# First head: row 1's turns and splits in another order; row 0 restacked first, expert weights in pieces

## The reference

```python
q_pool = q.reshape(B, H, S // 2, 2, D).mean(axis=3)        # B 2, H 8, S 1152, D 64
scores = (1.0 / np.sqrt(D)) * np.matmul(q_pool, k.transpose(0, 1, 3, 2))
scores = scores - np.max(scores, axis=-1, keepdims=True)
attn = np.exp(scores)
attn = attn / (np.sum(attn, axis=-1, keepdims=True) + 1e-09)
out = np.matmul(attn, v)

# x is attn_out as (1152, 512); 8 experts, each token goes to the one with the largest logit
h = np.maximum(x[mask] @ w1[e], 0.0)                        # w1 (8, 512, 1024)
out[mask] = gate_w[mask, None] * eom[mask, e, None] * (h @ w2[e])

h = x @ w_in                                                # w_in (512, 2048)
g = h * np.tanh(np.log1p(np.exp(h)))
return (g @ w_out).astype(np.float32)
```

## Time and profile before

| | |
|---|---|
| median of 3 runs | 677.72 us (677.46 to 678.32) |
| profiled execution | 679.0 us, of which the span shown is 677.3 |
| busy | PE 98%, DVE 75%, ACT 60%, POOL 14% |
| granted clock, mean | 0.998 |
| DMA | 93.83 MB, 139 GB/s over the span |

### The profile page before, as it was taken

One profiled execution on the slowest core, in us unless ns is written; L12 is line 12 of the kernel. 1 busy time (PEld: TensorE's weight loads), 2 busy tenths in 40 slices (PEclk: granted clock), 3 DMA queues, 4 the chain that ended last, 5 costly groups with the idle time before them and its releaser, 6 DMA issues.

```text
span 677.3 us, 14740 instructions
## 1 busy us (share of the span) xinstructions
PE 664.0 (98%) x5135; PEld 591.9 (87%) x5135; DVE 504.9 (75%) x1180; ACT 409.7 (60%) x839; POOL 92.0 (14%) x136
## 2 busy tenths in 40 slices
PE   8999999999999999999999999999999999999996
PEld 6889898988898999579999999899998988899995
DVE  5777677777777776676666676676999998887873
ACT  5767576666666666554656475666676655445542
POOL 7705040505041200220000000000000000101001
PEclk9999999999999999999999999999999999999999
DMA  8888869797977600469990752041200000001001
GB/s 182 186 274 211 249 146 259 181 261 176 264 172 204 150 2 9 174 244 395 398 367 16 279 199 83 15 156 54 86 1 1 1 0 1 32 16 47 1 0 47
DMA packets 95351, 93.83 MB, mean 139 GB/s; under 512 B 41920, under 2 KB 70976, under 8 KB 94784
## 3 DMA queue, kind: packets, MB, share of 16 engines
q1 hardware_dynamic: 91536, 84.39, 42.8%
q10 hardware_dynamic: 2320, 4.00, 1.9%
q0 software_dynamic: 1440, 4.72, 1.8%
HBM read 59.80 MB, written 16.78 MB: 113 GB/s over the span
## 4 chain that ended last, share of the span: by engine, by line
PE 81%; SPq 6%; DVE 5%; POOL 2%; issue 2%; ACT 2%; DMA 0%; ACTq 0%; DVEq 0%; POOLq 0%
PE score_banks L1161 14%; PE score_banks L1191 11%; PE score_banks L1176 10%; PE pvT L902 9%; PE turn L922 9%; PE score_banks L1213 4%; PE pvT L1213 4%; PE turn L1213 4%; PE score_banks L873 4%; PE score_banks L874 4%; SPq L560 2%; PE score_banks L879 1%; PE turn L823 1%; PE turn L1139 1%; PE turn L1148 1%
## 5 line engine op out<-in xcount | busy, mean ns | idle before, releaser
L1261 ACT ACTIVATE prob<-score_banks,nmax 128x1152 f32<-128x1152 f32 x72 | 88.0, 1222 | 51.8 <-DVE nmax L1527 51.8
L922 PE MATMUL turn<-ident,prob 128*128 128x128 f32 x648 | 102.4, 279 | 0.5 <-DVE probT L1583 0.5
L1161 PEld LDWEIGHTS score_banks<-xsT,w_slot 128*128 128x128 f32 x832 | 94.6, 192 | 2.2 <-issue 1.4
L1161 PE MATMUL score_banks<-xsT,w_slot 128*128 x832 | 95.2, 276 | 0.7 <-ACT xsT L1395 0.7
L1266 ACT ACTIVATE probT<-turn 128x384 f32<-128x384 f32 x144 | 69.9, 487 | 36.7 <-PE turn L922 36.7
L922 PEld LDWEIGHTS turn<-ident,prob 128*128 128x128 f32 x648 | 75.1, 141 | 15.0 <-issue 11.0
L902 PE MATMUL pvT<-probT,v_sb 128*64 128x128 f32 (+1 forms) x1404 | 85.9, 269 | 0.0
L902 PEld LDWEIGHTS pvT<-probT,v_sb 128*64 128x64 f32 x1404 | 69.5, 137 | 11.9 <-issue 11.9
L873 PE MATMUL score_banks<-kT,qT 128*128 128x384 f32 x192 | 70.7, 368 | 1.7 <-DMA kT<-k_lo 1.2
L1748 DVE TENSOR_TENSOR w_lo<-w_slot,w_hi 128x512 fp32r<-128x512 f32 x104 | 69.2, 689 | 3.3 <-ACT w_hi L1421 3.2
L1517 DVE TENSOR_REDUCE nmax_part<-score_banks 128x1 f32<-128x768 f32 x72 | 68.3, 949 | 2.0 <-PE score_banks L874 1.8
(11 more groups left out here) (261 smaller groups left out, 1332.8 us busy)
## 6 DMA issues: line engine op xcount, KB each, us to landing
w_slot<-moe_w SPq DMA_DIRECT2D x16, 2048.0 KB, 15.4
slots_dram<-zeros SPq DMA_DIRECT2D x8, 1472.0 KB, 11.6
raw_k<-k SPq DMA_DIRECT2D x16, 288.0 KB, 6.0
v_sb<-v SPq DMA_DIRECT2D x16, 288.0 KB, 4.6
w_in_sb<-moe_w_in SPq DMA_DIRECT2D x2, 2048.0 KB, 7.7
w_out_sb<-moe_w_out SPq DMA_DIRECT2D x2, 2048.0 KB, 9.3
raw_q<-q SPq DMA_DIRECT2D x14, 256.0 KB, 3.4
qT<-q_hi SPq DMA_DIRECT2D x28, 128.0 KB, 2.4
```

The lines of the kernel that those rows point to most:

```text
L922: last = pe.transpose(bank[:, j * P:(j + 1) * P], prob[:, s % 2, c * KC + j * P:c * KC + (j + 1) * P], ident[:, :])
L1161: last = pe.matmul(h1_bank[f % 4][:, 0:P], w1_e[:, d, f * P:(f + 1) * P], xsT[:, d, bass.ds((t % XS_RING) * P, P)], start=(d == 0), stop=( ...
L1261: act.activation(prob[:, s % 2, :].rearrange("p (c n) -> p c n", c=NC), scores[s % 2][:, :, 0:KC], ACT.Exp, bias=nmax[:, s:s + 1], accum_o ...
```

## The change

Four things are moved; two warming matmuls are removed. No other arithmetic is added or taken away.

1. TensorE, first head: the ninth tile's turn goes ahead of the second score product, the turns of row 1's keys go one place back, the query turns are halved around the first scores of tile 1, and the warming matmuls (`WARM_FIRST`) and two waits ahead of the loop go.
2. ScalarE and VectorE, first head: the copies follow the new order of turns, the one of the last key chunk goes behind the first exponential; VectorE splits the last queries of row 0 ahead of tile 1's first maximum.
3. GpSimd, first head: the first pair of row 1's queries is split ahead of the last key chunk; the step that reads a part waits for it by name.
4. SyncE: `restack` sends what row 0 needs first (four query DMAs, six key DMAs) and row 1 behind it; the expert weights go from between `restack(1)` and `load_kq(3)` to the ends of iterations 1, 2 and 3, one matrix each, the gates to that of iteration 4.

```diff
-        first_whole = [("k", 1, 1, 1), ("k", 1, 2, 2), ("q", 0, (FT, Q0), 3), ("k", 1, 0, 4), ("q", 1, (0, FT), 5)]
+        first_whole = [("q", 0, (FT, Q0), 1), ("k", 1, 1, 2), ("k", 1, 2, 3), ("k", 1, 0, 4), ("q", 1, (0, FT), 5)]
...
             def restack(h):
                 par = h % 2
                 sp.wait_ge(q_split, h)
-                for b in range(B):
...
+                restack_queries(0, par, 0, FT * P)
+                for c in range(NC):
+                    sp.wait_ge(k_split, NC * (h - 1) + c + 1)
+                    restack_keys(0, par, c * KC, KC)
+                restack_queries(1, par, Q0 * P, FT * P)
                 for var, q_part in enumerate((q_hi, q_lo)):
                     sp.dma_start(qT[:, par, var, FT * P:Q0 * P].bitcast(F32), q_part[:, FT * P:].bitcast(F32)
                                  ).then_inc(stacked[1], 16)
-                for c in range(NC):
-                    sp.wait_ge(k_split, NC * (h - 1) + c + 1)
-                    restack_keys(0, par, c * KC, KC)
                 restack_keys(1, par, 0, S)
...
             restack(1)
-            for n, w in enumerate((w_gate, w_ogate)):
...
-            load_expert(0, 0)
...
                 if h == 1:
-                    load_w1(1, 1)
+                    load_w1(0, 0)
                     sp.wait_ge(zeros_ready, 1)
                 else:
+                    if h == 2:
+                        load_w2(0, 0)
+                    elif h == 3:
+                        load_w1(1, 1)
+                    elif h == 4:
+                        load_gates()
                     for n in range(2 * (h - 2), min(2 * (h - 1), ZERO_PARTS)):
...
-            first_keys_split(WHOLE_CHUNK0, 3)
-            first_queries_split(WHOLE_Q, 4, (0, FT // 2))
-            first_queries_split(WHOLE_Q, 5, (FT // 2, FT))
-            first_queries_split(WHOLE_TAIL, 6, (FT, Q0))
+            first_queries_split(WHOLE_Q, SPLIT_PAIR0, 1, (0, FT // 2))
+            first_keys_split(WHOLE_CHUNK0, SPLIT_CHUNK0)
+            first_queries_split(WHOLE_Q, SPLIT_PAIR1, 2, (FT // 2, FT))
+            first_queries_split(WHOLE_TAIL, SPLIT_TAIL, 3, (FT, Q0))
...
             qk(0, 0)
+            first_tail()
+            pe.wait_ge(first_ready, FIRST_CHUNK2)
+            qk(0, 1)
             pe.wait_ge(first_k_landed[1], 16)
             whole_keys(1)
-            pe.wait_ge(first_ready, FIRST_CHUNK2)
-            qk(0, 1)
-            whole_keys(2)
             pe.wait_ge(first_ready, FIRST_CHUNK0)
             qk(0, 2)
-            first_tail()
+            whole_keys(2)
             whole_keys(0)
-            whole_queries()
+            whole_queries((0, FT // 2))
             pe.wait_ge(first_copied, WHOLE_CHUNK2)
             qk(1, 0)
-            pe.wait_ge(first_copied, WHOLE_TAIL)
             qk(1, 1)
-
-            pe.wait_ge(first_copied, WHOLE_CHUNK0)
-            for m in range(WARM_FIRST):
-                pe.matmul(turn[0][0:DH, 0:P], ident[:, 0:DH], ident[:, :], start=True, stop=True)
+            whole_queries((FT // 2, FT)).then_inc(whole_turned, 1)
             bodies(pe, pe_body)
...
-            for unit in first_units[:-1]:
+            for unit in first_units:
                 first_high(unit)
-            first_high(first_units[-1], (0,))
-            first_copy(first_whole[0])
-            first_high(first_units[-1], (1,))
-            for unit in first_whole[1:-1]:
-                first_copy(unit)
+            for n in (WHOLE_TAIL, WHOLE_CHUNK1, WHOLE_CHUNK2):
+                first_copy(first_whole[n - 1])
             exp(0, 0)
-            first_copy(first_whole[-1])
+            for n in (WHOLE_CHUNK0, WHOLE_Q):
+                first_copy(first_whole[n - 1])
             bodies(act, act_body)
...
             max_first(0, 0)
             max_rest(0, 0)
+            first_low(FIRST_CHUNK0)
             max_first(1, 1)
-            first_low(FIRST_CHUNK0)
             bodies(dve, dve_body)
```

More of the change, by code:

```diff
@@ L423, in build @@
         warm_bank = score_banks[:, 2, :]
-        WARM_BEFORE, WARM_BETWEEN, WARM_FIRST = 12, 3, 2
+        WARM_BEFORE, WARM_BETWEEN = 12, 3
         FIRST_Q, FIRST_TAIL = NC, NC + 1
@@ L586, in restack_keys, with restack_queries @@
                              ).then_inc(stacked[b], 16)
+            def restack_queries(b, par, at, n):
+                src = slice(b * DH, (b + 1) * DH)
+                for var in range(2):
+                    hi, lo = slice(var * DH, (var + 1) * DH), slice((1 - var) * DH, (2 - var) * DH)
+                    sp.dma_start(qT[hi, par, var, at:at + n].bitcast(F32), q_hi[src, 0:n].bitcast(F32)
+                                 ).then_inc(stacked[b], 16)
+                    sp.dma_start(qT[lo, par, var, at:at + n].bitcast(F32), q_lo[src, 0:n].bitcast(F32)
+                                 ).then_inc(stacked[b], 16)
             def restack(h):
@@ L620, in load_w2, with load_gates @@
                              ).then_inc(w_landed[n], 16)
+            def load_gates():
+                for n, w in enumerate((w_gate, w_ogate)):
+                    sp.dma_start(w_both[:, :, n * NE:(n + 1) * NE], w.rearrange("(t p) e -> p t e", p=P)
+                                 ).then_inc(wg_landed, 16)
             def load_expert(e, n):
@@ L706, in first_keys_split, with first_queries_split @@
                 pool.wait_ge(first_split, done)
-            def first_queries_split(n, done, tiles):
+            def first_queries_split(n, done, moved, tiles):
                 unit = ("q", first_whole[n - 1][1], tiles, 0)
@@ L716, in first_queries_split @@
                 pool.tensor_tensor(qT[here, 0, 1, cols], raw, high, ALU.subtract).then_inc(first_low_done, 1)
-                pool.wait_ge(first_low_done, done - SPLIT_KEYS)
+                pool.wait_ge(first_low_done, moved)
                 pool.tensor_copy(qT[there, 0, 1, cols], high).then_inc(first_moved, 1)
-                pool.wait_ge(first_moved, done - SPLIT_KEYS)
+                pool.wait_ge(first_moved, moved)
                 pool.tensor_copy(qT[there, 0, 0, cols], qT[here, 0, 1, cols].bitcast(F32)).then_inc(first_split, 1)
@@ L840, in first_queries, with whole_queries @@
                 last.then_inc(first_turned, 1)
-            def whole_queries():
-                for i in range(FT):
+            def whole_queries(tiles):
+                for i in range(*tiles):
                     last = pe.matmul(first_bank[FIRST_Q][DH:2 * DH, i * P:(i + 1) * P], q_pair[:, 0, i, 1, :], ident[:, :],
                                      start=True, stop=True)
-                last.then_inc(whole_turned, 1)
+                return last
             def first_tail():
@@ L947, in pe_body @@
                     pe.wait_ge(exp_done, g + 1)
+                    if first and s + 1 == FT:
+                        pe.wait_ge(first_split, SPLIT_CHUNK0)
                     if not (final and s == SB - 1):
@@ L1341, in first_high @@
                     act.wait_ge(first_ready, 1)
-                if 0 in parts:
-                    act.activation(qT[here, 0, 0, cols], src, ACT.Copy, scale=QS)
-                if 1 in parts:
-                    act.activation(qT[there, 0, 1, cols], src, ACT.Copy, scale=QS).then_inc(first_hi_ready, 1)
+                act.activation(qT[here, 0, 0, cols], src, ACT.Copy, scale=QS)
+                act.activation(qT[there, 0, 1, cols], src, ACT.Copy, scale=QS).then_inc(first_hi_ready, 1)
             def first_copy(unit):
```

14 lines of the change are left out of this document (6 added, 8 removed).

## The result

The changed kernel took 684.3 us (median of 4 executions, 682.09 to 684.77) against 678.02 for the kernel before on the same chip (4 executions, 677.46 to 679.63): a ratio of 1.0085, interval 1.007 to 1.010. The forecast was 680.0 with a range up to 682.3, so the direction was right and the size too small. The same kernel was measured twice more later (e1 and e12): 682.4, ratio 1.007 (1.0057 to 1.0082), and 681.95, ratio 1.006 (1.0043 to 1.0076). All 16 executions together have a median of 682.15 and run from 680.89 to 684.77; the first four were on the high side.

The account below looks back on a forecast made before the run. TensorE, busy 98%, was taken as the bound, so only its holes could move: - 0.9 - 1.5 + 1.2 + 3.4 + 0.1 = + 2.3 us on the profiled 679.0 is 681.3, less 1.3 for the median 680.0; range 675.3 to 682.3.

Parts of the forecast that it names:

- The first head: Reordered start on the compute engines: step 1 begins 0.9 us sooner, bounds 0.3 and 1.2.
- the splits: GpSimd's reordered splits in the first head: TensorE's cover stays, so they cost nothing.
- the wait ahead of head 2: TensorE's 1.22 us idle before head 2's first key product goes, a gain of 1.5 us with restart.
- the queue as the new bound: SyncE's DMA queue, with the weights in new places, brings keys for heads 4 and 5 later than TensorE asks.
- waits at heads 4 and 5: TensorE idles for keys 1.1 us ahead of head 4 and 3.3 ahead of head 5.
- the landing: Row 0's last key DMA lands 2.3 us after its issue, bounds 2.2 and 3.3.
- my sum of 681.3: Profiled execution of 679.0 us plus the terms' total of 2.3, before conversion to the median.
- the price of a matrix: A 2 MB expert matrix in SyncE's queue adds 5.6 us, bounds 5.2 and 6.1.
- rival B: No change: a matrix costs SyncE's queue only 3.9 to 4.9 us, giving 676.6 to 678.5; chance 0.22.
- Rival C: TensorE loses granted clock near head 5, in a hole of over 3 us, giving 683.6; chance 0.05.
- the high bounds: Matrix 6.1, long issue 0.6 and landing 3.3 together make the sum + 4.9 us.
- Long issues in restack 4: A first DMA issue into SyncE's full queue may take 1.22 instead of 0.60; half, 0.3 us, allowed.

Follow-up runs that it names:

- e1: The changed kernel again, no edit: 682.4 us, ratio 1.007.
- e12: The changed kernel a third time, no edit: 681.95 us, ratio 1.006.
- e8: The kernel before with only the new restack order, row 0 first, on SyncE: 677.5 us.
- e3: The changed kernel with gates and both expert matrices put back ahead of restack 2, the next behind it: 676.72 us, ratio 0.9983.
- e5: The changed kernel with the second and third matrix and the gates moved behind the last restack: 676.69 us, ratio 0.9984.
- e2: The kernel before with only the expert weights and gates in their new places: 683.98 us, ratio 1.0094.
- e4: The changed kernel with 12 transposes of the identity ahead of the wait for the first tile of heads 4 and 6: 684.24 us.
- e7: The kernel before with only the first head's new order on the four compute engines: 677.99 us.
- e10: The kernel of e9 with 14 transposes of the identity ahead of the wait for head 2's first tile: 681.69 us.
- e9: The kernel of e3 with the next matrix moved from behind restack 2 to ahead of it: 683.36 us.

## Why the prediction was wrong

**Right.** The first head (0.9 forecast, 0.8 by e8 less e3); the splits at no cost (e3); the wait ahead of head 2 gone; the queue as the new bound, with waits at heads 4 and 5 and none later; the landing (2.3, measured 2.2 between 135.15 and 137.34). Head 5 was to start at 172.4; the three profiles of the changed kernel have 173.42, 172.84 and 171.82, mean 172.7. The waits were to be 1.1 and 3.3; e1, whose clock stood, has 1.45 and 2.69. On the scale of the profiled execution my sum of 681.3 agrees with e1's 681.68. That it agrees so well is in part luck: the price of a matrix, 5.6, was too high (3.3 to 5.0 for the first, 3.9 to 4.4 for the second, in which rival B was right), and issues longer than allowed, below, made up for it.

**First wrong step: from the profiled execution to the median.** I took 1.3 off, since the profile of before was 1.3 above the median. But e8 points to what made that execution slow: the wait ahead of head 2, the very one that the change takes away and that I had just booked as a gain of 1.5. It was booked at more than the median execution loses to it. Starting from the median, 678.0, the gains are 0.8 and about 0.6 (e5: 676.69), and the cost of the holes with restarts is 4.9 (e1's span, 679.9, less 675.0 of e3): 681.5, not 680.0. Of these 1.5 us, 0.9 is the wait at head 2 (1.5 for 0.6), 0.3 the kernel before (678.02 for 677.72), 0.2 the holes (4.7 for 4.9) and 0.1 the first head.

**Second wrong step: the clock, put at nothing in the sum.** Rival C, a lost clock ahead of head 5, was right in kind, with a chance of 0.05 and the wrong condition, a hole of over 3 us, for which I had only the end of the trace and the 1.22 us hole to go by. There the last matmul ends at 671.16, and the clock falls from 1.00 to 0.50 within 674.00 to 675.00, at 674.4 by the mean of 0.72, which is 3.3 us behind it. Windows of the kernel before, TensorE alone:

```profile
671.00:674.00 3.00, 0.16 (x1) 1.00 0.45 175
674.00:675.00 1.00, 0.00 (x0) 0.72 0.68 262
675.00:677.00 2.00, 0.00 (x0) 0.50 0.00 0
```

By that very condition it belonged in my sum, which had a hole of 3.3. In the earlier trace rows no hole before the last slice moved the clock, the 1.22 at 72.50 among them, and I took that for cover up to 3. Nothing in the rows bounded it between 1.22 and 3.3. Over all profiles, the clock stood behind every hole up to 1.56 us (seven of them, 0.53 to 1.56) and fell by seven of the eight from 1.80 to 4.21, the exception being 2.69. What decides between 1.80 and 2.89, where it did both, was not found.

The stretch costs 1.5 behind head 5 (508.5 for 507.0). Behind head 4 it costs nothing that can be told, since the queue sets head 5's start: from head 4's start to head 5's are 36.08 with it and 36.05 (e12) and 35.55 (e1) without. So 681.5 becomes 683.0 where it falls behind head 5, and the 13 executions with a stretch have a median of 683.12. C's price was 3.6, a step of that length taken twice as long, where 1.5 was measured; its 683.6 is the nearest of my numbers to 684.3 for a loss that was under half as dear and far more frequent.

**The range** was too narrow by my own numbers: the high bounds, + 4.9 on 677.72, end at 682.6 and not at 682.3, and C's 683.6 was left outside it.

**A term too small.** Long issues in restack 4: 0.3 allowed, 1.45 found in the first profile (0.66 and 0.79 over 0.60), which with a shorter load of v (1.73 for 2.2) and its start 0.3 late makes the 1.05 by which heads 4 and 5 were late there. It is a spread more than a shift: e12 had its load of v 1.2 sooner, the matrix ahead issued in 0.59 instead of 2.19, and its hole at head 4 is 0.53. Part of that 0.59 is only moved: in e12 the key DMA ahead of the matrix took 1.39 instead of 0.60.

**Open.** The two steps lead to 681.5 to 683.0, with the pooled median of 682.15 between, and the first measurement's median is 684.3. No profile fell on an execution near 684.5, of which the first measurement had three. Half clock behind both holes, or a head 5 that starts near 174, would each give that. The mean clock of one of them, 0.993, means two stretches or a double one (one costs it 0.0025, and the profiled execution, with one, has 0.995); the other two have 0.995, and what they had was not seen. The measurements of the changed kernel were not all made on one chip, and that is not excluded as a cause either, though the kernel before has medians of 677.98 to 678.11 in every measurement. Why the queue takes 2.19 for the matrix's issue in one execution and 0.59 in another was not found.

## What to carry to other kernels

A wait seen in one profile may be that execution's own. Before its removal is booked, ask whether it is also why the profile is slower than the median, and book it once. A bulk load is priced by the slack of the place where it lands and by what the place before it has left over: here either of two equal matrices costs 0.5 to 1.5 us and both 5.5 with the slow stretches, while behind the last restack they cost nothing. And where a sum leaves TensorE idle for more than 1.5 us (here the clock stood behind 1.56 and fell by 1.80), add a chance of a slow stretch, and look whether the next wait pays it back.

## What the runs showed of the hardware

The half clock came in stretches of 3.41 us (six profiles: the first of the changed kernel, e2, e4, e7, e10 and e12; one of 6.83 in e9), and could begin after work had resumed: 1.0 us behind the end of the 1.80 us hole in the changed kernel, 1.4 us behind one of 2.45 in e2, but 1.2 us ahead of the end of 4.21 in e9. So the slow instructions need not stand next to the hole that brought them.

The same hole ahead of the same product differed by 1.3 us between three executions of one kernel (1.80, 1.45, 0.53), with the load of v for head 4 issued at 126.14, 126.27 and 124.92. And transposes of the identity that only fill a hole shortened the whole by 1.7 us in the median (e10, 681.69, for e9, 683.36).

A score product's row is longer than the distance to the next start: in the kernel before, the one at 72.78 has a row of 0.34, and the next starts at 72.95, 0.17 later.
